# One of 257 dimensions as an outer product on VectorE in place of a matmul, in a Fourier and two-MLP kernel

## The chip, the core and the metric

The kernel runs on one NeuronCore of a Trainium2 chip. The metric is the device time of one execution in microseconds (us). Its engines are called PE (TensorE, the matmuls), DVE (VectorE), ACT (ScalarE), POOL (GpSimd) and SP (SyncE, which issues most DMAs here). Each works through its own queue in order, and they meet at semaphores. Only PE writes matmul results; they go to PSUM, eight banks of 512 fp32 words per partition, which DVE and ACT read.

## What is computed

A two-dimensional Fourier transform over sequence and feature dimension, of which the real part is kept, then an MLP with squared ReLU, then one with a rational function:

```python
X = np.fft.fft(np.fft.fft(x, axis=1), axis=2).real      # x: 2 x 3008 x 256
x = X.reshape(6016, 256)
h = x @ w_in                                            # 256 x 2048
g = np.maximum(h, 0.0) ** 2
x = g @ w_out                                           # 2048 x 256
h = x @ w_in2
P = a[0] + a[1] * h + a[2] * h**2 + a[3] * h**3
Q = 1.0 + abs(b[0]) * abs(h) + abs(b[1]) * h**2
out = (P / (Q + 1e-06)) @ w_out2
```

## The kernel before

**Symmetry.** The input is real, so token k and token -k share their work. With the feature transform folded into w_in, h of token k is plus + minus and h of token -k is plus - minus. Plus needs 129 input dimensions (0 to 128) and minus 127, while a matmul takes 128. Plus has therefore one dimension too many, number 128, and minus one row free: the values of dimension 128 lie in row 0 of the second half (`y[...][0, 1, :]`), and the weights that belong to them in row 0 of the second half of the folded w_in.

**Precision.** Every fp32 value is split in a hi and a lo part (fp32r), and a product is three matmuls: lo of the weights by hi of the data, hi by lo, hi by hi. Dimension 128 takes a fourth matmul in plus (L828): `w_mid` and `y_mid` are full 128-row tiles of zeros with three rows set (hi, hi and lo of one operand against lo, hi and hi of the other), so that one matmul holds all three products.

**Stages.** Stage 1 (L745) is the first Fourier step; w_in is folded (L754), ACT keeps its hi (L478) and DVE its lo (L636). Stage 3 (L765) gives y, the transform of 256 token pairs at a time, in 12 tiles; ACT and DVE keep y_hi (L483) and y_lo (L640), SP stores them in DRAM and loads one tile at a time later (L363, with y_mid at L367). Ten of the 12 tiles are made before the main loop (`EARLY`), two in its first steps.

**The main loop.** A tile (256 pairs, 512 tokens; 196 pairs in the last) takes eight steps, each of two blocks of 128 of the 2048 hidden units; there are 96 steps. In step s PE does up1(s), that is minus (L817, six matmuls of 256 columns) and plus (L828, eight), then down1(s-2) (L802, twelve of 512 columns), up2(s-10) (L793, twelve) and down2(s-12) (L802, twelve). So the first ten steps have no second MLP, and steps behind the last up1 (from about 974 us) have only it.

- ACT in a step: relu and square (L501, L503), once a tile z_hi (L557), from h2 (L519, L527), the hi of g1 (L510), once a tile out_s (L564), abs of q (L533), the copy of minus for step s+1 (L495), ln and exp for a first reciprocal (L543, L546).
- DVE in a step: h = plus + minus and plus - minus (L658, L659), in the first eleven steps the lo of g1 (`split1`, L697), the division for the step before (L676, L678, L682), once a tile z_lo (`keep_z_lo`, L687), then from h2 (`read_h2`: L665, L666, L668). L665 waits for ACT's L527 of the same step. The next up2 on PE waits for L668 (`h2_read`), since both use the same two banks.
- POOL splits the weights w_out1, w_in2 and w_out2 (L421, L423; the last two at about 88 to 122 us), and from step 10 the g values (L446, L453, L455).

Plus stands in PSUM bank 0, minus in bank 1. PE's up1(m) waits for `diff_done` m, after which both banks are read.

## Time and profile before

| | |
|---|---|
| median of 3 runs | 1050.05 us (1049.68 to 1050.45) |
| profiled execution | 1051.58 us, span 1049.8 us |
| busy | PE 97%, DVE 84%, ACT 85%, POOL 54% |
| chain that ended last | PE 89%, DVE 6%, issue 3%, ACT 2% |
| mean granted TensorE clock | 0.989 of full speed |

Busy is the share of the span in which an engine had an instruction running; a matmul's length in a row includes the tail that overlaps the next, so the distance between starts is its price. A granted clock of 1.00 is 2.4 GHz and 0.50 is 1.2 GHz. A row of a timeline gives start and length in us, then engine, line, operation, output<-input and shapes; in brackets the idle time before it and what ended it.

### The profile page before, as it was taken

The page shows a single profiled execution, that of the slowest core. Times are in us where ns is not written, and L with a number is a line of the kernel's source. Part 1 is how long each engine was busy: PE and PEld are TensorE (multiplying, and loading weights), DVE is VectorE, ACT ScalarE, POOL GpSimd, SP SyncE. Part 2 cuts the span into 40 slices and gives each one's busy share as a digit, 9 for nine tenths or more (in the row PEclk, how much of TensorE's full clock was granted, in tenths as well). Part 3 has the DMA queues.
Part 4 walks back from the last instruction along what each step waited for, and adds up shares of the span by engine and source line. Part 5 has one row for each costly group of instructions (what it writes and reads, how often), then busy time and mean ns, then how long its engine had stood idle before and what let it go on. Part 6 is the DMA issues. An engine that isn't in the chain of part 4 may idle for free.

```text
span 1049.8 us, 13876 instructions
## 1 busy us (share of the span) xinstructions
PE 1021.1 (97%) x5288; PEld 868.6 (83%) x5288; DVE 884.0 (84%) x839; ACT 888.6 (85%) x929; POOL 570.6 (54%) x303
## 2 busy tenths in 40 slices
PE   9999999999999999999999999999999999999786
PEld 8798878888888888888888888888888888888675
DVE  2456888988988988888888888898898898898897
ACT  2348888999999999999999999999999998898683
POOL 0236765565665655655656556556566466466442
PEclk9999999999999999999999999999999999999897
DMA  9765000001001001001001001001001001000000
GB/s 249 282 205 193 1 1 21 1 1 41 1 1 42 1 1 41 1 1 41 2 1 41 1 1 41 1 1 41 1 1 41 1 1 36 1 21 2 0 21 16
DMA packets 22580, 36.50 MB, mean 35 GB/s; under 512 B 1601, under 2 KB 17394, under 8 KB 21874
## 3 DMA queue, kind: packets, MB, share of 16 engines
q1 hardware_dynamic: 22514, 35.63, 10.4%
q8 instruction: 41, 0.67, 0.3%
q14 instruction: 25, 0.20, 0.1%
HBM read 23.78 MB, written 11.81 MB: 34 GB/s over the span
## 4 chain that ended last, share of the span: by engine, by line
PE 89%; DVE 6%; issue 3%; ACT 2%; DMA 0%; SPq 0%; ACTq 0%; DVEq 0%
PE ps L802 45%; PE ps L793 23%; PE ps L828 8%; PE ps L817 6%; PE ps L745 3%; PE ps L765 2%; PE ps L754 1%; DVE w_out_unsplit_lo L665 1%; DVE den_s L665 1%; DVE w_out_unsplit_lo L678 1%; DVE w_out_unsplit_lo L676 1%; PE ps L772 1%; DVE w_in_unsplit_hi L666 1%; ACT g_value L527 0%; DVE w_in_unsplit_lo L666 0%
## 5 line engine op out<-in xcount | busy, mean ns | idle before, releaser
L802 PE MATMUL ps<-g_hi,w_out_lo 128*128 128x512 f32 (+1 forms) x764 | 300.9, 394 | 19.8 <-POOL w_in_hi L455 8.9
L802 PE MATMUL ps<-g_hi,w_out_hi 128*128 128x512 f32 (+1 forms) x764 | 299.9, 393 | 0.0
L802 PE MATMUL ps<-g_lo,w_out_hi 128*128 128x512 f32 (+1 forms) x728 | 283.3, 389 | 0.0
L453 POOL CAST g_hi<-g_value 128x1024 fp32r<-128x1024 f32 x86 | 89.7, 1043 | 349.1 <-DVE g_value L682 349.1
L455 POOL TENSOR_TENSOR g_lo<-g_value,g_hi 128x1024 fp32r<-128x1024 f32 x86 | 207.9, 2417 | 6.9
L446 POOL TENSOR_TENSOR g_lo<-g_value,g_hi 128x1024 fp32r<-128x1024 f32 (+1 forms) x86 | 203.8, 2370 | 1.3 <-ACT g_hi L510 1.3
L802 PEld LDWEIGHTS ps<-g_hi,w_out_lo 128*128 128x128 f32 x764 | 145.5, 190 | 49.4 <-POOL w_in_lo L455 10.2
L802 PEld LDWEIGHTS ps<-g_hi,w_out_hi 128*128 128x128 f32 x764 | 145.1, 190 | 29.3
L665 DVE SCALAR_TENSOR_TENSOR den_s<-den_s,b_abs,ps 128x1024 f32<-128x1024 f32 x88 | 112.7, 1281 | 62.4 <-ACT g_value L527 62.1
L802 PEld LDWEIGHTS ps<-g_lo,w_out_hi 128*128 128x128 f32 x728 | 137.6, 189 | 25.5
L676 DVE SCALAR_TENSOR_TENSOR den_s<-den_s,seed_s 128x1024 f32<-128x1024 f32 x87 | 110.9, 1275 | 28.7 <-ACT seed_s L546 28.7
L533 ACT ACTIVATE den_s<-den_s 128x1024 f32<-128x1024 f32 x88 | 93.5, 1063 | 38.4 <-DVE den_s L665 38.3
L793 PE MATMUL ps<-z_hi,w_in_lo 128*128 128x512 f32 (+1 forms) x384 | 118.8, 390 | 2.9 <-DVE g_value L668 2.7
L519 ACT ACTIVATE den_s<-ps,coef_s 128x1024 f32<-128x1024 f32 x88 | 98.2, 1116 | 24.4 <-PE ps L793 23.0
L793 PE MATMUL ps<-z_lo,w_in_hi 128*128 128x512 f32 (+1 forms) x384 | 117.5, 387 | 0.0
L793 PE MATMUL ps<-z_hi,w_in_hi 128*128 128x512 f32 (+1 forms) x384 | 117.3, 387 | 0.0
L682 DVE SCALAR_TENSOR_TENSOR g_value<-g_value,coef_s,den_s 128x1024 f32<-128x1024 f32 x86 | 110.5, 1285 | 3.0
L668 DVE SCALAR_TENSOR_TENSOR g_value<-g_value,coef_s,ps 128x1024 f32<-128x1024 f32 x86 | 110.1, 1281 | 3.0
L678 DVE SCALAR_TENSOR_TENSOR den_s<-den_s,seed_s 128x1024 f32<-128x1024 f32 x87 | 106.6, 1225 | 3.0
L501 ACT ACTIVATE g_value<-g_value 128x1024 f32<-128x1024 f32 (+1 forms) x96 | 100.1, 1042 | 8.2 <-DVE g_value L659 8.2
L666 DVE TENSOR_TENSOR g_value<-g_value,ps 128x1024 f32<-128x1024 f32 x86 | 104.4, 1214 | 0.0
L527 ACT ACTIVATE g_value<-ps,coef_s 128x1024 f32<-128x1024 f32 x86 | 103.3, 1201 | 0.0
(99 smaller groups left out, 1882.8 us busy)
## 6 DMA issues: line engine op xcount, KB each, us to landing
x_s<-x SPq DMA_DIRECT2D x16, 384.0 KB, 7.0
out_t<-out_s SPq DMA_DIRECT2D x11, 512.0 KB, 3.1
w_out_unsplit_lo<-w_out SPq DMA_DIRECT2D x2, 2048.0 KB, 18.2
tw_s<-twiddle SPq DMA_DIRECT2D x1, 3012.0 KB, 17.8
y_hi_dram<-y_stage_hi SPq DMA_DIRECT2D x10, 256.0 KB, 3.2
y_lo_dram<-y_stage_lo SPq DMA_DIRECT2D x10, 256.0 KB, 3.5
y_hi<-y_hi_dram SPq DMA_DIRECT2D x10, 256.0 KB, 2.8
y_lo<-y_lo_dram SPq DMA_DIRECT2D x10, 256.0 KB, 3.1
```

The lines of the kernel that those rows point to most:

```text
L446: nc.gpsimd.tensor_tensor(g1_lo_s[:, p, :, 0:n], r_s[:, p, :, 0:n], g1_hi_s[:, m % 2, :, 0:n].bitcast(F32), ALU.subtract).then_inc(pool_lo ...
L455: nc.gpsimd.tensor_tensor(lo, g, hi.bitcast(F32), ALU.subtract).then_inc(g2_lo, 1)
L501: nc.scalar.activation(r, r, ACT.Relu).then_inc(relu_done, 1)
L527: nc.scalar.activation(num_of(m), h2_banks(m)[:, :, 0:width(m)], ACT.Identity, bias=a2, scale=a3).then_inc(cubic_done, 1)
L665: nc.vector.scalar_tensor_tensor(den, den, b_abs[:, 0:1], h2, ALU.add, ALU.mult).then_inc(q_signed, 1)
L666: nc.vector.tensor_tensor(num, num, h2, ALU.mult).then_inc(t_h_done, 1)
L668: nc.vector.scalar_tensor_tensor(num, num, a1, h2, ALU.add, ALU.mult).then_inc(h2_read, 1)
L676: nc.vector.scalar_tensor_tensor(den, den, Q_CONST, seed, ALU.add, ALU.mult).then_inc(t_done, 1)
L678: nc.vector.scalar_tensor_tensor(den, den, 2.0, seed, ALU.subtract, ALU.mult, reverse0=True).then_inc(rec_done, 1)
L682: nc.vector.scalar_tensor_tensor(num, num, a0, den, ALU.add, ALU.mult).then_inc(g2_done, 1)
L793: last = nc.tensor.matmul(h[:, i, 0:n], lhs, rhs, start=(j == 0), stop=(j == len(products) - 1))
L802: last = nc.tensor.matmul(acc[:, mb, 0:n], w[a][:, f, mb * P:(mb + 1) * P], g[c][:, i, 0:n], start=(f == 0 and j == 0), stop=(f == FB - 1 ...
```

## The change

Dimension 128 leaves the matmuls of plus. DVE writes the outer product of its 256 y values (the same row in all partitions, `u_s`) and its 128 weights (one per partition, a column of `w_col`) into bank 0, two instructions per step with `tensor_scalar`, and PE's six remaining matmuls of plus accumulate on it (`start=False` throughout). `outer_product(s + 1)` stands in DVE's step s behind the division and z_lo and ahead of `read_h2`; the first stands ahead of the loop. PE's plus waits for `outer_ready`, two per step. PE's minus now waits for `minus_kept` where up1 waited for `diff_done`.

For the operands: the row of y is copied by DVE from PSUM with each y_lo (`u_stage`, ahead of the y_lo subtraction), stored in DRAM by SP and loaded by SP into all partitions, in two buffers a tile ahead. The weight row goes from SBUF to DRAM (SP) and back as 32 rows (ACT issues that load at the fourth early tile); PE adds hi and lo and turns them to columns with one small matmul behind the ten early stages 3, and DVE copies the result. The memsets of `w_mid` and `y_mid`, the three DMAs of `w_mid` and three per tile of `y_mid` are gone.

```diff
@@ SP
+            after(sp, s1_ready, S1_GROUPS)
+            sp.dma_start(pair_s[:, :], pair).then_inc(pair_loaded, 16)
-            def load_mid(t, hi, lo):
-                for row, v in enumerate((hi, hi, lo)):
-                    sp.dma_start(y_mid[row:row + 1, 0:pairs(t)].bitcast(F32), v).then_inc(y_mid_loaded, 16)
+            def store_u(t):
+                n = t % (STAGE_BUFS + 1)
+                sp.wait_ge(u_kept, t + 1)
+                sp.dma_start(u_d[:, t * WIDE:t * WIDE + pairs(t)], u_stage[:, n, 0:pairs(t)]).then_inc(u_stored[n], 16)
+
+            def load_u(t):
+                n = pairs(t)
+                after_u_stored(sp, t)
+                sp.dma_start(u_s[:, t % U_BUFS, 0:n], u_d[:, t * WIDE:t * WIDE + n].to_broadcast([P, n])
+                             ).then_inc(u_loaded[t % U_BUFS], 16)
-            sp.wait_ge(mid_zeroed, 2)
             sp.wait_ge(w_in1_lo, folds)
-            for row, n in enumerate((1, 0, 0)):
-                sp.dma_start(w_mid[row:row + 1, :].bitcast(F32), w_in1_s[n][0:1, 1, :].bitcast(F32)).then_inc(w_mid_loaded, 16)
-            sp.wait_ge(y_lo_kept, 1)
-            load_mid(0, *(s[0:1, 1, :].bitcast(F32) for s in y_s))
+            for n in range(2):
+                sp.dma_start(w_row_d[n:n + 1, :], w_in1_s[n][0:1, 1, :].bitcast(F32)).then_inc(w_row_stored, 16)
+            store_u(0)
             for t in range(1, TILES):
+                store_u(t)
                 store_y(t)
+                if t <= U_BUFS:
+                    load_u(t - 1)
@@ SP, main loop
                 load_y(t)
-                load_mid(t, *(v[0:1, 1, t * WIDE:t * WIDE + pairs(t)] for v in y_d))
+                if t + 1 < TILES and t + 1 >= U_BUFS:
+                    load_u(t + 1)
@@ ACT
             for t in range(EARLY):
                 keep_y_hi(t)
+                if t == MID_AT:
+                    act.wait_ge(w_row_stored, 32)
+                    act.dma_start(w_rows[:, :], w_row_d.rearrange("n (f p) -> (n f) p", p=P)).then_inc(w_rows_loaded, 16)
@@ DVE
-            dve.memset(w_mid[:, :].bitcast(F32), 0.0).then_inc(mid_zeroed, 1)
-            dve.memset(y_mid[:, :].bitcast(F32), 0.0).then_inc(mid_zeroed, 1)
             def keep_y_lo(t):
                 hi, lo = y_tile(t)
                 dve.wait_ge(y_hi_kept, t + 1)
+                if t > STAGE_BUFS:
+                    after_u_stored(dve, t - STAGE_BUFS - 1)
+                nc.vector.tensor_copy(u_stage[:, t % (STAGE_BUFS + 1), 0:pairs(t)], uv_bank(t)[0:1, 1, :]).then_inc(u_kept, 1)
@@
                 if t == MID_AT:
-                    dve.wait_ge(w_mid_loaded, 48)
+                    dve.wait_ge(w_row_stored, 32)
@@
+            dve.wait_ge(w_col_summed, 1)
+            nc.vector.tensor_copy(w_col[:, :], ps[:, FOLD_BANKS[2], 0:FB]).then_inc(w_col_ready, 1)
+            dve.wait_ge(w_col_ready, 1)
+
+            def outer_product(m):
+                t, n = m // UNITS, pairs(m // UNITS)
+                if m % UNITS == 0:
+                    dve.wait_ge(u_loaded[t % U_BUFS], 16 * (t // U_BUFS + 1))
+                after(dve, diff_done, m)
+                for i in range(2):
+                    f = 2 * (m % UNITS) + i
+                    nc.vector.tensor_scalar(h1_plus(m)[:, i, :], u_s[:, t % U_BUFS, 0:n], w_col[:, f:f + 1], None, ALU.mult
+                                            ).then_inc(outer_ready, 1)
@@
+            outer_product(0)
             for s in range(STEPS):
@@
                     keep_z_lo(summed // UNITS)
+                if unit(s + 1) is not None:
+                    outer_product(s + 1)
                 if second is not None:
                     read_h2(second)
@@ PE
             for t in range(EARLY):
                 stage3(t)
+            pe.wait_ge(pair_loaded, 16)
+            pe.wait_ge(w_rows_loaded, 16)
+            nc.tensor.matmul(ps[:, FOLD_BANKS[2], 0:FB], w_rows[:, :], pair_s[:, :], start=True, stop=True
+                             ).then_inc(w_col_summed, 1)
@@ PE, up1
-                after(pe, diff_done, m)
+                after(pe, minus_kept, m)
@@
-                if m % UNITS == 0:
-                    pe.wait_ge(y_mid_loaded, 48 * (t + 1))
+                pe.wait_ge(outer_ready, 2 * m + 2)
                 for i in range(2):
                     f = slice((2 * (m % UNITS) + i) * P, (2 * (m % UNITS) + i + 1) * P)
-                    products = [(w_in1_s[1][:, 0, f], y_s[0][:, 0, 0:n]), (w_in1_s[0][:, 0, f], y_s[1][:, 0, 0:n]),
-                                (w_mid[:, f], y_mid[:, 0:n]), (w_in1_s[0][:, 0, f], y_s[0][:, 0, 0:n])]
-                    for j, (lhs, rhs) in enumerate(products):
-                        last = nc.tensor.matmul(h1_plus(m)[:, i, :], lhs, rhs, start=(i == 0 and j == 0), stop=(j == 3),
-                                                skip_group_check=True)
+                    for a, c in ((1, 0), (0, 1), (0, 0)):
+                        last = nc.tensor.matmul(h1_plus(m)[:, i, :], w_in1_s[a][:, 0, f], y_s[c][:, 0, 0:n],
+                                                start=False, stop=(a, c) == (0, 0), skip_group_check=True)
```

## Rows read from the trace of the kernel before

**Rows 1.** Busy time by stretch: stretch, length, PE PEld DVE ACT POOL, clock, DMA, GB/s.
```profile
350.30:429.90 79.60, 79.58 (x402) 67.37 (x401) 70.39 (x66) 73.20 (x75) 46.66 (x24) 1.00 0.04 14
906.00:974.00 68.00, 67.17 (x358) 59.12 (x357) 60.60 (x57) 59.51 (x64) 37.69 (x22) 1.00 0.02 9
```

**Rows 2.** Chain that ended last, in order of time: start, us, what.
```profile
113.73 0.95 PE ps L828 x8
...
145.17 4.41 PE ps L793 x12
...
355.99 2.98 PE ps L793 x12
...
435.63 3.00 PE ps L793 x12
...
950.23 2.74 PE ps L793 x12
...
959.38 2.74 PE ps L793 x12
```

**Rows 3.** Timeline of DVE, one step of the steady part.
```profile
401.02 1.28 DVE L665 SCALAR_TENSOR_TENSOR den_s<-den_s,b_abs,ps 128x1024 f32<-128x1024 f32 x1 [0.91 <-ACT g_value L527]
...
403.47 1.28 DVE L668 SCALAR_TENSOR_TENSOR g_value<-g_value,coef_s,ps 128x1024 f32<-128x1024 f32 x1
404.67 0.68 DVE L658 TENSOR_TENSOR g_value<-ps,minus_s 128x512 f32<-128x512 f32 x1
405.27 0.68 DVE L659 TENSOR_TENSOR g_value<-ps,minus_s 128x512 f32<-128x512 f32 x1
406.22 1.23 DVE L676 SCALAR_TENSOR_TENSOR den_s<-den_s,seed_s 128x1024 f32<-128x1024 f32 x1 [0.27 <-ACT seed_s L546]
...
408.75 1.28 DVE L682 SCALAR_TENSOR_TENSOR g_value<-g_value,coef_s,den_s 128x1024 f32<-128x1024 f32 x1
410.94 1.28 DVE L665 SCALAR_TENSOR_TENSOR den_s<-den_s,b_abs,ps 128x1024 f32<-128x1024 f32 x1 [0.91 <-ACT g_value L527]
```

**Rows 4.** Timeline of PE, the first matmul of plus and the first behind it.
```profile
401.94 0.28 PE L828 MATMUL ps<-y_hi,w_in_lo 128*128 128x256 f32 x1
...
402.88 0.39 PE L802 MATMUL ps<-g_hi,w_out_lo 128*128 128x512 f32 x1
```

**Rows 5.** Timeline of ACT in the same step.
```profile
402.34 1.06 ACT L533 ACTIVATE den_s<-den_s 128x1024 f32<-128x1024 f32 x1 [0.49 <-DVE den_s L665]
```

**Rows 6.** Timeline of DVE, z_lo and the operation behind it.
```profile
114.33 1.23 DVE L687 TENSOR_TENSOR z_lo<-ps,z_hi 128x1024 fp32r<-128x1024 f32 x1
115.47 0.68 DVE L658 TENSOR_TENSOR g_value<-ps,minus_s 128x512 f32<-128x512 f32 x1
```

**Rows 7.** Timeline of DVE at the start of the main loop.
```profile
68.51 0.69 DVE L640 TENSOR_TENSOR y_stage_lo<-ps,y_stage_hi 128x512 fp32r<-128x512 f32 x1 [1.10 <-ACT y_stage_hi L483]
...
75.84 1.23 DVE L697 TENSOR_TENSOR g_lo<-g_value,g_hi 128x1024 fp32r<-128x1024 f32 x1
76.98 0.56 DVE L640 TENSOR_TENSOR y_stage_lo<-ps,y_stage_hi 128x392 fp32r<-128x392 f32 x1
```

**Rows 8.** Timeline of PE, first matmul of plus in steps 0 and 2.
```profile
68.39 0.28 PE L828 MATMUL ps<-y_hi,w_in_lo 128*128 128x256 f32 x1
...
76.06 0.28 PE L828 MATMUL ps<-y_hi,w_in_lo 128*128 128x256 f32 x1
```

**Rows 9.** Instructions of L697 (split1): length in ns min/median/max, first and last start.
```profile
L697 DVE TENSOR_TENSOR g_lo<-g_value,g_hi x10: 1212/1855/3323, 75.8 to 116.7; 128x1024 fp32r<-128x1024 f32 x10
```

**Rows 10.** Timeline of PE, the longest idle time of the first 900 us.
```profile
145.17 0.73 PE L793 MATMUL ps<-z_hi,w_in_lo 128*128 128x512 f32 x2 [1.91 <-DVE g_value L668]
```

**Rows 11.** Busy time of PE by stretch, shortly after: stretch, length, PE, clock, DMA, GB/s.
```profile
147.00:149.00 2.00, 2.00 (x7) 0.50 0.00 0
```

**Rows 12.** Timeline of DVE, L665 in steps 10 and 11.
```profile
122.61 1.28 DVE L665 SCALAR_TENSOR_TENSOR den_s<-den_s,b_abs,ps 128x1024 f32<-128x1024 f32 x1 [3.75 <-ACT g_value L527]
...
132.00 1.28 DVE L665 SCALAR_TENSOR_TENSOR den_s<-den_s,b_abs,ps 128x1024 f32<-128x1024 f32 x1 [0.40 <-ACT g_value L527]
```

More of the change, by code:

```diff
@@ L48 @@
 MID_AT = 3
+U_BUFS = 2
 WIDE = 2 * BATCH * N2
@@ L179, in kept_and_rest @@
             return value, sb(f"{name}_lo", [P, bufs, 2, TN], F32R)
-        w_mid = sb("w_mid", [P, DFF], F32R)
-        y_mid = sb("y_mid", [P, WIDE], F32R)
+        u_s = sb("u_s", [P, U_BUFS, WIDE])
+        w_rows = sb("w_rows", [2 * FB, P])
+        pair_s = sb("pair_s", [2 * FB, FB])
+        w_col = sb("w_col", [P, FB])
+        u_stage = sb("u_stage", [1, STAGE_BUFS + 1, WIDE])
+        sb("to_w_in2", [P, DFF + WIDE - (U_BUFS + STAGE_BUFS + 1) * WIDE - P - 2 * FB])
         w_in2_s, (_, w_in2_raw) = weights("w_in2", [P, DB, DFF])
@@ L875, in _ @@
             pe.wait_ge(w_in1_lo, folds)
-            pe.wait_ge(w_mid_loaded, 48)
             pe.wait_ge(mid_row_zeroed, 2)
```

17 lines of the change are left out of this document (13 added, 4 removed).

## The prediction

> **What bounds the kernel now.** I read the table of busy time by stretch first. From 350.3 to 429.9 us, one tile of eight steps, PE is busy for 79.58 of 79.60 us at full clock, DVE for 70.39 and ACT for 73.20; the last h1 tile (906 to 974) looks alike [rows 1]. So PE sets the pace, and a tile lasts 435.63 - 355.99 = 79.64 us [rows 2]. Matmuls taken off PE shorten the time only until another engine comes last, so what counts is how near DVE is. The timeline of one step shows it: DVE's L665 starts at 401.02 and again at 410.94, a step of 9.92 us, and DVE is idle twice in it, 0.27 us before L676 and 0.91 us before L665, both times for ACT [rows 3]. The new DVE work falls just into the 0.91.
>
> **PE's side.** In plus the eight matmuls (L828) take 402.88 - 401.94 = 0.94 us, 0.118 each [rows 4]. Two fewer per step is -0.236: a step needs 9.68 us of PE, a tile 79.64 - 1.89 = 77.75. The 96 steps hold 22.6 us of it, the most the change can give.
>
> **What a product costs DVE.** No row of before shows DVE writing PSUM, nor this operation. Nearest rows: L658, 512 columns, gives way to L659 after 0.60 us, that is 512 columns at 1.04 ns (from 512 to 1024 columns an element costs (1.28 - 0.68)/512 to 1.04 ns depending on form) plus 0.07. L668, with a per-partition scalar read from memory, is 1.28 long and gives way after 1.20 = 1.07 + 0.13; L676, whose scalars are constants, is only 1.23 long [rows 3]. The product reads such a scalar (a column of w_col), so I take 0.27 + 0.13 = 0.40 us of DVE per product of 256 columns and 0.48 to its end: 0.80 per step, 0.88 until PE may go on. Lower bound 0.27 (two elements at a time, the same 0.13), middle 0.34 (scalar for nothing), upper 0.50 (a dearer write to PSUM).
>
> By the Trainium skill, "VectorE: DVE Perf Modes", section "The TRN2 errata", a lone fp32 operation of N elements takes (N+151)/0.96 ns, an estimate of 424 ns here; less the 0.08 overlap that would be the 0.34 of the first rival. The trace agrees with it for L658 (0.68) and not for the forms with a scalar from memory (1.28 for 1024, where it gives 1.22).
>
> **The steady loop.** L665 starts, ACT's L533 follows 1.32 later, then L495, L543 and L546, whose end releases DVE's L676 at 406.22 [rows 3, 5]: 5.20 us. L676 and L678 take 408.75 - 406.22 = 2.53 together, and L682 gives way after 1.20, as L668 does: 8.93. In before the next L665 then waits for L527. In after, outer_product(s+1) stands there: 8.93 + 0.80 = 9.73, above PE's 9.68. The 0.91 cover is used up. Once a tile z_lo (L687) stands in this place as well. It gives way after 115.47 - 114.33 = 1.14 us [rows 6], so this step takes 10.87. A tile: 8 x 9.73 + 1.14, and 0.2 for ACT's out_s and for POOL overlap (estimate) = 79.1. The gain per tile is 0.5 and not 1.89. From 152 to 906 us are 9.5 tiles: **-4.5 us** (at 0.27: -18, PE-bound; at 0.34: -14.5; at 0.50, the loop at 9.93: +10).
> What is late next: PE's plus of the step after z_lo waits for outer_ready about 1 us. Queued behind it on PE are down1, up2 and down2, for which ACT and DVE wait; since the loop is DVE's, that wait is the same time seen on PE.
>
> **The last h1 tile.** With 196 columns a product is 0.34, and the loop 5.1 (a narrower L495) + 3.73 + 0.67 = 9.5, against steps of 959.38 - 950.23 = 9.15 [rows 2]. Seven steps: **+2**.
>
> **The first ten steps.** There is no h2 work here; a step of PE is up1 and down1. Three things come on:
> (a) outer_product(0). The product of step 0 must wait for PE's w_col matmul, which itself stands behind the last early stage 3, for the y_lo copy that starts at 68.51 [rows 7] and now has a row copy of u before it (0.34), for a copy of w_col (about 0.2) and for itself (0.88): 70.5. Its plus started at 68.39 [rows 8]: 2.1 us later.
> (b) step 2. On DVE in step 1 come y_lo(10), split1(0) at 75.84, y_lo(11) at 76.98 [rows 7] and only then outer_product(2). Two u copies add 0.6, the end of y_lo(11) is near 78.1, the product 79.0, and with the delay of (a) passed on less 0.24 and some slack 80.5. Plus(2) ran at 76.06 [rows 8]: +4.4. PE is in order, so down1(0) is late by the same.
> (c) a new loop through steps 3 to 10: plus(s) 0.71 and 0.2 to its reader, add and subtract 1.20, split1(s-1), outer_product(s+1) 0.88, plus(s+1): 2.98 plus the length of split1. That length goes from 1.21 (median 1.86) to 3.32 us [rows 9], long while POOL splits the second weights. So I take 4.2, 4.2, 4.5, 4.75, 5.0, 5.0, then 6.3, and 7.4 with z_lo behind the last: 41.4 us from plus(2) to plus(10). Before it was 113.73 - 76.06 = 37.67 [rows 2, 8]: +3.7.
> Together +8.1, less 0.2 for the shorter plus(10): **+7.9**. Bounds 4 (POOL's splits end before the late steps, slack in step 1) and 10.
> (d) the clock. After an idle time of 1.91 us at 145.17 the granted clock of the stretch 147 to 149 is 0.50, the 1.2 GHz level [rows 10, 11]; the twelve matmuls took 4.41 where 2.74 is usual [rows 2], 1.67 lost. Waits of over 2 us will stand ahead of plus(0), plus(2) and plus(10). Three times 1.67 less what is hidden: **+3.5**, bounds 0 and 5.
> (e) steps 10 to 12 are paced by the loop of ACT and DVE already, at 132.00 - 122.61 = 9.39 us [rows 12]: 9.73 makes **+1**.
>
> **At nothing.** The two memsets and the 39 small DMAs (3 of w_mid, 36 of y_mid) that go lie beside waits of others. Added on SP: two stores of w_row, twelve stores and twelve loads of u, and pair. The loads of u are a tile ahead, so a landing has most of a tile, 80 us, as cover; without that DVE's product would wait for it once a tile. The first u and the way of w_row through DRAM start with the first early tiles and have until 68, some 10 us. The u stores stand before y's stores on SP, a short issue each; the load of w_in2 follows y_lo(11), some 2 us later, and POOL's splits with it. On ACT the load of w_rows waits for w_row_stored at step 3 of the early tiles and may hold up y_hi a little. PE's minus now waits for minus_kept, earlier than diff_done. The tail after 974 us, DVE's chain, isn't touched and only starts later.
>
> **Sum.** -4.5 + 2 + 7.9 + 3.5 + 1 = +9.9 us. The profiled execution took 1051.58 (span 1049.8), 1.5 above the median of 1050.05; added to the median this is **1060**.
>
> **Rivals.**
> First: a product costs 0.34. Then a tile takes 8 x 9.60 + 1.3 = 78.1: -14.5, last tile +1, head 7 + 3.5 + 0.5: -2.5, about 1047.5. For it: plain forms cost 0.07 beyond their elements. Against: every form here with a scalar from memory is dearer. 0.2.
> Second: DVE has room and PE stays the bound (a product of 0.27 or less), as the change says. -18, +0.5, +6.5 and +3: -8, 1042. The row that speaks for it is DVE's 70.39 of 79.60 busy; against it speaks the loop through ACT, which busy shares don't show. 0.1.
> Third: the head loses little, since the waits of steps 1 to 10 overlap others, at 0.40 per product: -4.5 + 2 + 1 and 3: 1051.5, the same. 0.1.
> Fourth, slower still: the wait of about 1 us behind z_lo is enough to halve the clock each tile. 1.67 lost, 0.7 of it hidden, 9.5 times 1: 1069.5. It decides from where idle is as long as the 1.91 us there [rows 10]. 0.1.
> The forecast has 0.5.
>
> **How the numbers follow.** 0.2% (2.1 us) is about what a measurement can tell from no change. Faster is the second rival and most of the first; no change is the third and the rest of the first; slower the forecast and the fourth: 0.25, 0.15, 0.6. The range leaves out the tip of either side: 1044 to 1068; the forecast's own, from its bounds, is 1053 to 1067.
>
> **What would show it.** Products of 0.48 us each, giving way after 0.40; L665 in steady steps behind outer_product and not behind L527; steps of 9.7; PE idle once a tile ahead of plus; plus(0) near 70.5, plus(2) near 80.5, plus(10) near 122; a clock of 0.5 in parts of 70 to 90. The forecast is wrong if products take 0.35, if PE is still busy without gaps past 152 us, or if plus(10) comes before 118.

## The result

The changed kernel takes 1053.88 us (median of 8 runs, 1052.88 to 1055.89), the kernel before 1050.65 (8 runs), a ratio of 1.0029 with an interval of 1.0020 to 1.0038. It is slower by 3.2 us; the forecast was slower by about 10.

| | before | after |
|---|---|---|
| profiled execution, span | 1051.58, 1049.8 us | 1054.85, 1053.1 us |
| first matmul of minus, step 0 | 67.60 | 67.61 |
| read_h2 of step 10 | 122.61 | 134.00 |
| second z_lo | 190.88 | 203.04 |
| last but one z_lo | 907.46 | 910.56 |
| last z_lo | 975.84 | 980.12 |
| busy | PE 97%, DVE 84%, ACT 85%, POOL 54% | PE 96%, DVE 89%, ACT 84%, POOL 54% |

The table says where the time went: 11.4 us are lost ahead of step 10 and 0.8 up to the second z_lo, 9.1 come back between the second and the last but one z_lo (907.46 - 190.88 = 716.58, now 707.52), 1.2 are lost in the last h1 tile and 1.0 comes back behind it: 3.3 in the two spans. In the kernel after, line numbers have moved: L665, L666 and L668 of read_h2 are L709, L710 and L712 now, L676, L678 and L682 of the division L720, L722 and L726, z_lo is L731, split1 L741, the products are L693, and on PE plus is L876, minus L868, down L853, up2 L844, stage 3 L812. DVE's subtract is L703. On ACT L524 keeps minus, L572 and L575 are the ln and the exp ahead of the division, L556 is the second of the two that read h2, L586 is z_hi.

The page of after: busy time, and the chain that ended last by engine and by line.

```profile
PE 1009.3 (96%) x5098; PEld 852.9 (81%) x5098; DVE 941.7 (89%) x1042; ACT 882.0 (84%) x929; POOL 569.5 (54%) x303
DVE 45%; ACT 28%; issue 14%; PE 12%; DMA 0%; DVEq 0%; ACTq 0%; SPq 0%
```

PE's share of the chain went from 89% to 12% while its busy share fell by one point only. The steady stretch of [rows 1], of after, and two from the start (stretch, length, busy of PE PEld DVE ACT POOL, clock, DMA, GB/s):

```profile
67.50:115.50 48.00, 42.56 (x231) 36.95 (x231) 32.18 (x53) 32.77 (x39) 23.49 (x12) 0.89 0.48 164
115.50:152.00 36.50, 28.75 (x128) 23.83 (x127) 25.41 (x31) 26.31 (x28) 17.73 (x9) 0.86 0.00 0
350.30:429.90 79.60, 78.99 (x390) 66.39 (x389) 76.58 (x84) 73.45 (x76) 47.11 (x25) 1.00 0.05 16
```

In the steady stretch PE is idle 0.6 us of 79.60, and no more. That another path is nevertheless a bound is seen in the chain, here one step of it (start, us, what):

```profile
408.70 1.28 DVE g_value L726
409.99 0.79 DVE ps L693 x2
410.77 1.20 DVE den_s L709
...
412.96 0.58 ACT minus_s L524
413.54 1.05 ACT seed_s L572
...
414.61 1.17 ACT seed_s L575
...
415.87 1.24 DVE den_s L720
417.13 1.24 DVE den_s L722
418.39 0.03 DVE g_value L726
```

From L726 to L726 it is a closed loop through DVE and ACT with no matmul in it, and the two products lie in it. Its length is 418.39 - 408.70 = 9.69 us. The timeline of DVE shows the same step as [rows 3]:

```profile
409.90 0.87 DVE L693 TENSOR_SCALAR ps<-u_s,w_col 128x256 f32<-128x256 f32 x2
410.68 1.27 DVE L709 SCALAR_TENSOR_TENSOR den_s<-den_s,b_abs,ps 128x1024 f32<-128x1024 f32 x1
...
415.87 1.23 DVE L720 SCALAR_TENSOR_TENSOR den_s<-den_s,seed_s 128x1024 f32<-128x1024 f32 x1 [0.27 <-ACT seed_s L575]
...
420.38 1.27 DVE L709 SCALAR_TENSOR_TENSOR den_s<-den_s,b_abs,ps 128x1024 f32<-128x1024 f32 x1
```

The 0.91 us ahead of L665 have gone and the 0.27 ahead of the division have stayed. The pair of products gives way after 410.68 - 409.90 = 0.78. In this tile (351 to 430 us) the distances of L709 are seven times 9.68 to 9.70 and, in the step with z_lo, 10.81; 7 x 9.69 + 10.82 is the usual tile of 78.65. PE's wait for the products over the whole steady part (in total, times, longest) is small, one per tile, behind z_lo:

```profile
PE ps L876 <- DVE ps L693: 5.4, 9, 0.7
```

The start, on PE: first matmuls of plus in steps 0, 2 and 10, and stage 3 behind the first.

```profile
70.08 0.38 PE L876 MATMUL ps<-y_hi,w_in_lo 128*128 128x256 f32 x1 [1.50 <-DVE ps L693]
...
71.27 3.16 PE L812 MATMUL ps<-tw_s,s_s 128*128 128x128 f32 x16
...
81.52 0.58 PE L876 MATMUL ps<-y_hi,w_in_lo 128*128 128x256 f32 x1 [3.16 <-DVE ps L693]
...
123.58 0.38 PE L876 MATMUL ps<-y_hi,w_in_lo 128*128 128x256 f32 x1 [3.08 <-DVE ps L693]
```

Plus of step 0 is 1.7 us later than in [rows 8], plus of step 2 is 5.5 later, plus of step 10 10.0 later than the 113.56 at which the timeline of before has it. ([rows 2] show 113.73 for it, but that row is of the chain, where a group of matmuls begins when the tail of the one ahead has ended.) In front of the last one ACT and DVE did this (ACT first):

```profile
120.48 1.00 ACT L586 ACTIVATE z_hi<-ps 128x1024 fp32r<-128x1024 f32 x1
```
```profile
121.52 1.22 DVE L731 TENSOR_TENSOR z_lo<-ps,z_hi 128x1024 fp32r<-128x1024 f32 x1 [2.01 <-ACT z_hi L586]
122.66 0.86 DVE L693 TENSOR_SCALAR ps<-u_s,w_col 128x256 f32<-128x256 f32 x2
```

ACT's z_hi needs the sums of PE's down1, whose last matmul ends at 119.78, and stands in ACT's queue behind the relu and square of step 9, which came from PE's plus and end at 120.58. DVE's z_lo waits 2.01 us for z_hi, the product of step 10 is queued behind z_lo, and PE's plus waits 3.08 us for the product. A product whose place is behind an operation that waits for PE's results makes PE wait for itself. And behind this wait the twelve matmuls of down1 took 4.34 us where the twelve of up2 behind them take 2.77; the chain has them, and the clock of the stretch is 0.50:

```profile
124.56 4.34 PE ps L853 x12
128.89 2.77 PE ps L844 x12
```
```profile
125.50:127.50 2.00, 2.00 (x6) 1.53 (x5) 2.00 (x4) 1.49 (x2) 0.00 (x0) 0.50 0.00 0
```

PE's longest wait for a product, 4.51 us ahead of plus at 143.84, comes behind this part, and the clock is 0.50 from 143 to 147 us. It costs nothing of its own here: from L709 at 134.00 to L709 at 164.70 the chain has no matmul, only DVE and ACT.

### The profile page after: what moved, and what is told of

Same layout as the page of the kernel before. It is cut to its first block, busy times and chain, and to the rows that moved or that the text cites. A ratio compares the mean times of both kernels' runs of the same rounds, so it can differ in the third digit from the quotient of the medians.

```text
span 1053.1 us, 13706 instructions
## 1 busy us (share of the span) xinstructions
PE 1009.3 (96%) x5098; PEld 852.9 (81%) x5098; DVE 941.7 (89%) x1042; ACT 882.0 (84%) x929; POOL 569.5 (54%) x303
## 4 chain that ended last, share of the span: by engine, by line
DVE 45%; ACT 28%; issue 14%; PE 12%; DMA 0%; DVEq 0%; ACTq 0%; SPq 0%
ACT seed_s L575 9%; DVE den_s L709 9%; DVE den_s L722 9%; DVE den_s L720 9%; ACT seed_s L572 8%; DVE g_value L726 8%; ACT minus_s L524 5%; DVE ps L693 4%; PE ps L853 3%; PE ps L792 3%; PE ps L812 2%; PE ps L801 1%; ACT g_value L556 1%; DVE z_lo L731 1%; PE ps L844 1%
## 5 line engine op out<-in xcount | busy, mean ns | idle before, releaser
L853 PE MATMUL ps<-g_hi,w_out_lo 128*128 128x512 f32 (+1 forms) x764 | 302.2, 396 | 18.1 <-POOL w_in_hi L481 8.2
L853 PE MATMUL ps<-g_hi,w_out_hi 128*128 128x512 f32 (+1 forms) x764 | 301.3, 394 | 0.0
L853 PE MATMUL ps<-g_lo,w_out_hi 128*128 128x512 f32 (+1 forms) x728 | 285.3, 392 | 0.0
L853 PEld LDWEIGHTS ps<-g_hi,w_out_lo 128*128 128x128 f32 x764 | 146.9, 192 | 47.0 <-POOL w_in_lo L481 9.5
L853 PEld LDWEIGHTS ps<-g_hi,w_out_hi 128*128 128x128 f32 x764 | 146.3, 191 | 29.8
L853 PEld LDWEIGHTS ps<-g_lo,w_out_hi 128*128 128x128 f32 x728 | 138.8, 191 | 25.9
L720 DVE SCALAR_TENSOR_TENSOR den_s<-den_s,seed_s 128x1024 f32<-128x1024 f32 x87 | 106.8, 1228 | 25.5 <-ACT seed_s L575 25.5
L844 PE MATMUL ps<-z_hi,w_in_lo 128*128 128x512 f32 (+1 forms) x384 | 118.9, 391 | 1.8 <-DVE g_value L712 1.8
L709 DVE SCALAR_TENSOR_TENSOR den_s<-den_s,b_abs,ps 128x1024 f32<-128x1024 f32 x88 | 111.9, 1272 | 8.6 <-ACT g_value L556 8.3
L844 PE MATMUL ps<-z_lo,w_in_hi 128*128 128x512 f32 (+1 forms) x384 | 117.2, 386 | 0.0
L844 PE MATMUL ps<-z_hi,w_in_hi 128*128 128x512 f32 (+1 forms) x384 | 116.9, 386 | 0.0
L726 DVE SCALAR_TENSOR_TENSOR g_value<-g_value,coef_s,den_s 128x1024 f32<-128x1024 f32 x86 | 110.5, 1284 | 3.0
L712 DVE SCALAR_TENSOR_TENSOR g_value<-g_value,coef_s,ps 128x1024 f32<-128x1024 f32 x86 | 110.2, 1281 | 3.0
L722 DVE SCALAR_TENSOR_TENSOR den_s<-den_s,seed_s 128x1024 f32<-128x1024 f32 x87 | 106.6, 1225 | 3.0
L710 DVE TENSOR_TENSOR g_value<-g_value,ps 128x1024 f32<-128x1024 f32 x86 | 104.3, 1213 | 0.0
L556 ACT ACTIVATE g_value<-ps,coef_s 128x1024 f32<-128x1024 f32 x86 | 103.1, 1198 | 0.0
```

What stands on the lines that cost most here:

```text
L556: nc.scalar.activation(num_of(m), h2_banks(m)[:, :, 0:width(m)], ACT.Identity, bias=a2, scale=a3).then_inc(cubic_done, 1)
L709: nc.vector.scalar_tensor_tensor(den, den, b_abs[:, 0:1], h2, ALU.add, ALU.mult).then_inc(q_signed, 1)
L710: nc.vector.tensor_tensor(num, num, h2, ALU.mult).then_inc(t_h_done, 1)
L712: nc.vector.scalar_tensor_tensor(num, num, a1, h2, ALU.add, ALU.mult).then_inc(h2_read, 1)
L720: nc.vector.scalar_tensor_tensor(den, den, Q_CONST, seed, ALU.add, ALU.mult).then_inc(t_done, 1)
L722: nc.vector.scalar_tensor_tensor(den, den, 2.0, seed, ALU.subtract, ALU.mult, reverse0=True).then_inc(rec_done, 1)
```

## The experiments

Unless it says otherwise an experiment is an edit of the changed kernel. Ratios are to the kernel before, run on the same chip; that kernel's median was 1051.17 beside e1, e2, e3 and e4_head_place, 1050.16 beside e4b to e7 and 1051.20 beside e8 to e12. The diffs show the lines that matter and not each line of an edit. Head means the time from the first matmul of minus(0) to read_h2 of step 10: 55.01 us before, 66.39 after. Tile is the usual distance of two z_lo in the steady part: 79.64 before, 78.65 after. Last is the distance of the last two z_lo: 68.38 before, 69.56 after.

| | median us | ratio (95%) | head | tile | last |
|---|---|---|---|---|---|
| e1_six_matmuls | 1034.11 | 0.9838 (0.9824 to 0.9853) | 52.57 | 78.06 | 67.95 |
| e2_constant_scalar | 1048.98 | 0.9978 (0.9969 to 0.9988) | 65.70 | 78.18 | 68.88 |
| e9_four_halves | 1076.95 | 1.0246 (1.0226 to 1.0266) | 65.73 | 80.54 | 71.01 |
| e5_eight_matmuls | 1067.35 | 1.0165 (1.0149 to 1.0180) | 67.84 | 79.72 | 69.79 |
| e3_early_place | 1038.62 | 0.9882 (0.9867 to 0.9897) | 57.96 | 78.07 | 67.89 |
| e4_head_place | 1044.84 | 0.9945 (0.9930 to 0.9960) | 56.57 | 78.65 | 69.54 |
| e4b_steady_place | 1047.39 | 0.9972 (0.9961 to 0.9983) | 66.46 | 78.06 | 67.96 |
| e8_step1_only | 1050.20 | 0.9993 (0.9984 to 1.0003) | 61.22 | 78.65 | 69.58 |
| e11_early_column | 1051.40 | 1.0007 (0.9998 to 1.0017) | 64.18 | 78.65 | 69.55 |
| e6_filler | 1051.54 | 1.0013 (1.0003 to 1.0024) | 60.70 | 78.65 | 69.58 |
| e12_changed_again | 1054.03 | 1.0030 (1.0018 to 1.0041) | 64.92 | 78.65 | 69.58 |
| e7_both_ends | 1033.81 | 0.9845 (0.9831 to 0.9860) | 53.27 | 78.06 | 67.96 |

### What the shorter PE alone is worth

An edit of the kernel before: the matmul of w_mid and y_mid is left out and nothing takes its place, so dimension 128 is missing from h of the first layer.

```diff
-                                (w_mid[:, f], y_mid[:, 0:n]), (w_in1_s[0][:, 0, f], y_s[0][:, 0, 0:n])]
+                                (w_in1_s[0][:, 0, f], y_s[0][:, 0, 0:n])]
```

> The PE half of the change alone: the kernel before without its fourth matmul in plus, so dimension 128 is left out of the first MLP, and with no product on DVE. Theory (PE sets the pace before the change, and DVE's product is what takes the gain back): the full saving of 0.236 us per step appears, a tile goes from 79.64 to 77.75, L665 stays behind L527, the head gains about 2 us and the last tile 1.5: 1050.6 - 22 = 1029 us. Rival (PE was not the only bound, another loop holds the step near 9.7): a tile stays near 78.6 and the time near 1040.

Measured: 17.1 us faster, not the 22.6 of the 192 matmuls. The tile is 78.06 and not 77.75, and the last tile 67.95, only 0.43 shorter. PE's waits between 160 and 900 us, a kind that the kernel before doesn't have there:

```profile
PE ps L793 <- DVE g_value L668: 3.3, 10, 1.0
```

That is 0.33 us per tile, 0.25 in most: in the step with z_lo up2 waits for DVE's read_h2, and this is most of the 78.06 - 77.75. So even without a product PE isn't alone in setting the pace, and the ceiling of the change lay at 17 us; the 1029 us expected were too low, and a tile of 78.6 as the rival had it didn't come. PE's own step without the two matmuls is seen here too, from the starts of minus in three steps (z_lo comes between the last two):

```profile
413.57 0.28 PE L817 MATMUL ps<-y_hi,w_in_lo 128*128 128x256 f32 x1
...
423.26 0.28 PE L817 MATMUL ps<-y_hi,w_in_lo 128*128 128x256 f32 x1
...
433.44 0.28 PE L817 MATMUL ps<-y_hi,w_in_lo 128*128 128x256 f32 x1
```

The usual step is 9.69 and the one with z_lo 10.18. The usual step of the changed kernel is 9.69 as well. So the products cost nothing in seven steps of eight, and what after lacks against this ceiling, 78.65 - 78.06, stands in the step with z_lo alone, 10.82 against 10.18. In the last tile the steps keep the length that they had before; PE's busy 67.17 of 68.00 [rows 1] had looked like a bound and wasn't one.

### How long the loop is

Three kernels change the DVE work in the loop, or PE's, by a known amount. In the first the column of w_col is a constant, so that dimension 128 has wrong weights:

```diff
-                    nc.vector.tensor_scalar(h1_plus(m)[:, i, :], u_s[:, t % U_BUFS, 0:n], w_col[:, f:f + 1], None, ALU.mult
+                    nc.vector.tensor_scalar(h1_plus(m)[:, i, :], u_s[:, t % U_BUFS, 0:n], 0.5, None, ALU.mult
```

> The changed kernel with the constant 0.5 in place of the column of w_col, so dimension 128 has wrong weights; place and number of the products are unchanged. Theory (the loop L709, L524, L572, L575, L720, L722, L726, two products sets the steady step at 9.69; a scalar from memory costs 0.06 us): a product gives way after 0.33 instead of 0.39, the loop falls to 9.57, below PE's 9.68, a tile goes from 78.65 to between 77.8 and 78.1, the last tile gains 1: 1045 to 1047 us. Rival 1 (the scalar costs nothing): products and time as in the changed kernel, 1053.9. Rival 2 (PE's handshake with DVE, not the length of the loop, holds the step): product shorter, but tile still 78.6.

DVE of this kernel:

```profile
427.04 0.75 DVE L693 TENSOR_SCALAR ps<-u_s 128x256 f32<-128x256 f32 x2
427.69 1.27 DVE L709 SCALAR_TENSOR_TENSOR den_s<-den_s,b_abs,ps 128x1024 f32<-128x1024 f32 x1
...
432.88 1.31 DVE L720 SCALAR_TENSOR_TENSOR den_s<-den_s,seed_s 128x1024 f32<-128x1024 f32 x1 [0.27 <-ACT seed_s L575]
```

The pair gives way after 0.65 instead of 0.78, a product after 0.33: the scalar from memory costs 0.06 each. DVE's steps went to 9.64 only, since L720 takes 1.31 here instead of 1.23 and so takes 0.08 of the 0.13 back; behind z_lo it takes 1.23, and there the step is 9.57. (When this L720 starts, a subtraction of POOL that began at 430.68 still has 0.23 us to run; in after it is 0.10. The last section comes back to this.) PE's steps stay at 9.69, their length without any product, except in the step with z_lo, where they went from 10.75 to 10.33: DVE, now a little faster than PE in the usual steps, makes up for part of z_lo there. The tile is 78.18 and not 78.1 or less, the time 1048.98 and not 1045 to 1047 as expected. A product of 0.33 is the first rival's price, and its tile was 78.1.

In the second each product is made in two halves:

```diff
-                    nc.vector.tensor_scalar(h1_plus(m)[:, i, :], u_s[:, t % U_BUFS, 0:n], w_col[:, f:f + 1], None, ALU.mult
-                                            ).then_inc(outer_ready, 1)
+                    for part in (slice(0, n // 2), slice(n // 2, n)):
+                        nc.vector.tensor_scalar(h1_plus(m)[:, i, part], u_s[:, t % U_BUFS, part], w_col[:, f:f + 1], None, ALU.mult
+                                                ).then_inc(outer_ready, 1)
@@ PE
-                pe.wait_ge(outer_ready, 2 * m + 2)
+                pe.wait_ge(outer_ready, 4 * m + 4)
```

> The changed kernel with each product written as two halves of 128 columns, so four short instructions a step in the same place; nothing is left out. Theory (the loop through DVE and ACT is the steady step, to the last tenth): a half gives way after 0.25 us (0.13 for its elements and 0.12 fixed, the rest of 0.39), four take 1.02 instead of 0.78, a step goes from 9.69 to 9.93 and a tile from 78.65 to 80.6: +18 in the steady part, +1.7 in the last tile, +2 in the head: 1076. Rival (the step is set by something else with slack for DVE of 0.2 us or more): 1056 or less.

```profile
435.50 1.11 DVE L694 TENSOR_SCALAR ps<-u_s,w_col 128x128 f32<-128x128 f32 x4
436.52 1.27 DVE L710 SCALAR_TENSOR_TENSOR den_s<-den_s,b_abs,ps 128x1024 f32<-128x1024 f32 x1
```

The four give way after 1.02, which is 0.24 more than the pair, and a step is 9.93, 0.24 more than 9.69; the tile is 1.89 longer, about eight times 0.24. What is added to DVE in this place is added to the step in full: the loop has no slack left. What is taken off does not all come back, as e2_constant_scalar showed, since PE's own step is as long.

In the third the hi by lo matmul is issued twice per block, so its product counts twice, and PE has eight matmuls in plus again:

```diff
-                    for a, c in ((1, 0), (0, 1), (0, 0)):
+                    for a, c in ((1, 0), (0, 1), (0, 1), (0, 0)):
```

> The DVE half of the change alone: the changed kernel with two matmuls per step more in plus (w_hi by y_lo twice, so that term counts double), which gives PE its old 9.92 us per step. Theory: DVE's loop of 9.69 lies below PE's 9.92, so the products cost nothing in steady steps: tiles of 79.6 to 79.7 as in the kernel before, no wait of PE for L693 there. The head keeps its loss and adds PE's 0.24 per step: L709 of step 10 near 135.5. The last tile (loop 9.46 against PE's 9.15) loses 1.2. Sum: 1050.7 + 13 = 1064. Rival (DVE's writes to PSUM or the handshake slow PE by themselves): tiles above 80 and 1068 or more.

The steady stretch of this kernel:

```profile
350.30:429.90 79.60, 79.60 (x401) 67.49 (x400) 76.11 (x81) 73.14 (x74) 46.66 (x24) 1.00 0.05 16
```

PE is busy throughout, waits for nothing between 160 and 900 us, and the tile is 79.72 against 79.64 before. At PE's step of 9.93 the products are free. How z_lo is paid for is seen in L709, here behind a step with z_lo of 10.90:

```profile
366.02 1.28 DVE L709 SCALAR_TENSOR_TENSOR den_s<-den_s,b_abs,ps 128x1024 f32<-128x1024 f32 x1
...
375.72 1.27 DVE L709 SCALAR_TENSOR_TENSOR den_s<-den_s,b_abs,ps 128x1024 f32<-128x1024 f32 x1
```

The next steps of DVE are 9.70, 9.69, 9.77 and 9.85 and then PE's 9.93 again: the loop runs at its own 9.69 until it has made up for z_lo. In after it can't, since PE's step has come down to the loop's. So the change gained PE's 0.23 in the usual steps and lost the cover for z_lo: 79.64 - 78.65 = 0.99 per tile in place of 1.89. Of the 17 us that this kernel is slower than before, 12.8 are the head and 1.4 the last tile; 1064 was expected.

### The place of the products

The products of step s+1 need that add and subtract of step s have read bank 0, and nothing else that is late. In the next kernel they stand directly behind it.

```diff
                 add_and_subtract(s)
+                if unit(s + 1) is not None:
+                    outer_product(s + 1)
...
-                if unit(s + 1) is not None:
-                    outer_product(s + 1)
                 if second is not None:
                     read_h2(second)
```

> The changed kernel with outer_product(s+1) directly behind add_and_subtract(s) in every step, where DVE waits 0.27 us for L575 anyway; nothing is left out. Theory (loops): in steady steps the pair hides 0.27 us and costs 0.5 to 0.6 in the loop, which falls to 9.4 to 9.5, below PE's 9.68: tile 77.75 to 77.9, L709 behind L556 again. In the head the product no longer stands behind split1, y_lo and z_lo: plus(2) near 78 instead of 81.5, one halving of the clock less, L709 of step 10 at 124 to 126 instead of 134.0. Together 1050.6 + 2.5 - 18 - 2 = 1033 us. Rival (DVE is simply full, 76.6 of 78.65 us busy per tile, or PE pays for accumulating on a bank that DVE wrote): a tile stays within 0.3 of 78.65, and only the head's part of 8 to 9 us comes: 1045.

```profile
433.26 0.68 DVE L703 TENSOR_TENSOR g_value<-ps,minus_s 128x512 f32<-128x512 f32 x1
433.98 0.87 DVE L693 TENSOR_SCALAR ps<-u_s,w_col 128x256 f32<-128x256 f32 x2
434.76 1.22 DVE L720 SCALAR_TENSOR_TENSOR den_s<-den_s,seed_s 128x1024 f32<-128x1024 f32 x1
...
437.27 1.28 DVE L726 SCALAR_TENSOR_TENSOR g_value<-g_value,coef_s,den_s 128x1024 f32<-128x1024 f32 x1
438.47 1.28 DVE L709 SCALAR_TENSOR_TENSOR den_s<-den_s,b_abs,ps 128x1024 f32<-128x1024 f32 x1
```

The products now begin in the gap in which the division waited for ACT, so 0.27 of them is free, L709 stands directly behind L726, and this step behind z_lo is 9.45. In the others L720 takes up to 1.42 and a step of DVE is about 9.65, still under PE's 9.69. A tile is 78.07, the same as in e1_six_matmuls, where there is no product at all. The kernel is faster than before by 1.2%, 12.6 us; 1033 us had been expected, from tiles of 77.75 to 77.9 that e1_six_matmuls doesn't reach either. The next two make this move in the first ten steps only, and from step 10 on only (the diff of the first; the second has the two conditions the other way round):

```diff
+                if s < SKEW:
+                    outer_product(s + 1)
...
-                if unit(s + 1) is not None:
+                if s >= SKEW and unit(s + 1) is not None:
                     outer_product(s + 1)
```

> The changed kernel with the product directly behind add_and_subtract in steps 0 to 9 only; from step 10 on it stands where the changed kernel has it. Theory (the head costs 11.4 us by the start of the second MLP, of which 1.7 are the late first product and 8 to 10 the place of the others and the clock they cost): L709 of step 10 at 124 to 126, tiles 78.65 as in the changed kernel: 1044 to 1046 us. Rival (the head's delay is made up later in any case, since the chain's later parts have slack): the time stays at 1053, with the tail or the tiles longer.

> The changed kernel with the product directly behind add_and_subtract from step 10 on, and in its old place before. Theory: the steady part and the last tile gain what e3 gained there, 0.59 per tile (78.65 to 78.06) and 1.3: 5.4 + 1.3 less 0.9 that the tail gave back = 1048. L709 of step 10 near 134 as in the changed kernel. Rival (the head's lag and the steady loop interact): tiles near 78.65 again.

Each against the kernel before on its own chip, the head alone is at -6.3 us, the steady part alone at -2.8 and both at -12.6, where the changed kernel is at +3.2. So the moves gave 9.6, 6.0 and 15.8, and the parts add up (15.6). Beside the 6.0 stand 0.59 per tile over some nine tiles and 1.6 in the last h1 tile; beside the 9.6 a head that is 9.8 shorter.

### What the head is made of

First the product of step 2 alone, the only one placed early:

```diff
+                if s == 1:
+                    outer_product(s + 1)
...
-                if unit(s + 1) is not None:
+                if s != 1 and unit(s + 1) is not None:
                     outer_product(s + 1)
```

> The changed kernel with only the product of step 2 moved: in DVE's step 1 it stands directly behind add_and_subtract, ahead of y_lo(10), split1(0) and y_lo(11). Theory: plus(2) starts near 78.3 instead of 81.5 and the clock isn't halved in 81 to 85 us, so L709 of step 10 comes at 129 instead of 134.0, and the time is 1049.5. The other 4 to 5 us that e4 gained are then those of steps 3 to 10, behind split1 and z_lo. Rival (all of it belongs to steps 3 to 10): L709 of step 10 at 133 or later, 1053.

Then the other cause at the start, the late w_col. PE's matmul for it stands behind the eighth of the ten early stages 3, and DVE's copy and the product of step 0 behind the eighth y_lo; all else is as in after:

```diff
+COL_AT = 7
...
@@ DVE, behind keep_y_lo(t) of the early tiles
+                if t == COL_AT:
+                    dve.wait_ge(w_col_summed, 1)
+                    nc.vector.tensor_copy(w_col[:, :], ps[:, FOLD_BANKS[2], 0:FB]).then_inc(w_col_ready, 1)
+                    dve.wait_ge(w_col_ready, 1)
+                    outer_product(0)
@@ PE, behind stage3(t)
+                if t == COL_AT:
+                    pe.wait_ge(pair_loaded, 16)
+                    pe.wait_ge(w_rows_loaded, 16)
+                    nc.tensor.matmul(ps[:, FOLD_BANKS[2], 0:FB], w_rows[:, :], pair_s[:, :], start=True, stop=True
+                                     ).then_inc(w_col_summed, 1)
```

> The changed kernel with only the start moved: the w_col matmul behind the eighth early stage 3, its copy and the product of step 0 behind y_lo(7). Theory: plus(0) at 68.2 instead of 70.1 and no halved clock in 71 to 73 us, so everything to step 10 comes 1.7 to 3.3 us earlier, L709 of step 10 at 131 to 132, time 1051. Rival (step 2's wait takes it up): L709 of step 10 at 134, time 1053.9.

And the changed kernel once more beside these two:

> The changed kernel unchanged, beside the others on the same chip, as the measure for them and for how far two executions differ in the head. Every theory: 1053 to 1055, L709 of step 10 at 133 to 135, tiles 78.65.

Against the changed kernel on the same chip (1054.03, head 64.92), the early product of step 2 alone gives 3.8 us (head -3.7) and the early w_col alone 2.6 us, with a head only 0.7 shorter, though plus(0) starts 0.79 us behind minus(0) as before and not 2.47 as in after; the profiled execution of e11_early_column (1053.67) is the slowest of its ten, so its median is the better witness. The rest of the head, from e8_step1_only's 61.22 to e4_head_place's 56.57, is 4.7 us: the products of steps 3 to 10, which stood behind split1 and, in step 10, behind z_lo. e8_step1_only still has PE's 3.08 us of idle time ahead of plus(10), while in e4_head_place no wait for a product is over 0.5 us from plus(1) to plus(10). How the rest is shared among the other steps isn't shown.

### The clock

The idle times of 1.50 and 3.16 us in the head are followed in after by the lower level of the clock, as in [rows 10, 11]. Here 11 and 22 extra matmuls into an unused bank fill them, so that PE isn't idle; they take nothing from what follows them unless they are too many; of the two idle times 0.17 and 0.67 us are left.

```diff
                 last.then_inc(minus_ready, 1)
+                for _ in range({0: 11, 2: 22}.get(m, 0)):
+                    nc.tensor.matmul(ps[:, FOLD_BANKS[3], 0:WIDE], w_in1_s[0][:, 0, 0:P], y_s[0][:, 0, :], start=True, stop=True)
                 pe.wait_ge(outer_ready, 2 * m + 2)
```

> The changed kernel with 11 matmuls of 256 columns into an unused bank ahead of PE's wait for the products of step 0 and 22 ahead of that of step 2, so that PE isn't idle there. Theory (these two idle times of 1.5 and 3.2 us halve the granted clock, 0.50 in 71 to 73 and 81 to 85 us, and that costs 3 us): clock 1.00 through 68 to 90, the sixteen stage 3 matmuls behind plus(0) take 1.8 instead of 3.4 us, L709 of step 10 at 131 instead of 134.0, time 1051. Rival (the clock's loss lies beside other waits): clock 1.00 but L709 of step 10 stays at 134 and the time at 1053.9.

PE of this kernel; then PE of e12_changed_again, that is of after in another execution; then the clock between 71 and 73 us in after, in this kernel and in e12_changed_again.

```profile
68.99 1.48 PE L873 MATMUL ps<-y_hi,w_in_hi 128*128 128x256 f32 x11
70.65 0.39 PE L878 MATMUL ps<-y_hi,w_in_lo 128*128 128x256 f32 x1 [0.17 <-DVE ps L693]
...
71.47 1.95 PE L812 MATMUL ps<-tw_s,s_s 128*128 128x128 f32 x16
```
```profile
70.84 0.39 PE L876 MATMUL ps<-y_hi,w_in_lo 128*128 128x256 f32 x1 [1.50 <-DVE ps L693]
...
71.66 1.95 PE L812 MATMUL ps<-tw_s,s_s 128*128 128x128 f32 x16
...
80.89 0.39 PE L876 MATMUL ps<-y_hi,w_in_lo 128*128 128x256 f32 x1 [3.31 <-DVE ps L693]
...
82.17 0.62 PE L853 MATMUL ps<-g_hi,w_out_hi 128*128 128x512 f32 x1
```
```profile
71.00:73.00 2.00, 2.00 (x12) 2.00 (x11) 1.46 (x3) 0.11 (x1) 0.00 (x0) 0.50 1.11 332
```
```profile
71.00:73.00 2.00, 2.00 (x20) 2.00 (x19) 1.30 (x3) 0.00 (x0) 0.00 (x0) 1.00 1.11 340
```
```profile
71.00:73.00 2.00, 2.00 (x19) 2.00 (x20) 1.14 (x2) 0.00 (x0) 0.00 (x0) 1.00 1.11 331
```

With the gaps filled the sixteen matmuls of stage 3 took 1.95 us, in after 3.16. But the same 1.50 us of idle time ahead of them brought the lower level in one execution of the changed kernel and not in the other. And the filled kernel kept the full clock at a place that wasn't filled, ahead of plus(10); here that wait and the eight us behind it:

```profile
119.98 0.39 PE L878 MATMUL ps<-y_hi,w_in_lo 128*128 128x256 f32 x1 [3.09 <-DVE ps L693]
```
```profile
121.00:129.00 8.00, 8.00 (x42) 6.76 (x41) 3.55 (x6) 4.58 (x5) 4.82 (x3) 1.00 0.00 0
```

So the clock's share of the head isn't one number, and the filled kernel's profiled execution owes part of its head to a place without filler. That head is 5.7 us shorter than that of after, while the median is 1.4 us above the kernel before on its chip, where after was 3.2 and e12_changed_again 2.8 above. How much of the 11.4 us a clock that stays up would give back in a typical execution is settled no better than this, from 1.4 to 5.7 us.

### Both together

The early place for all products, as in e3_early_place, and the early w_col, as in e11_early_column:

```diff
+COL_AT = 7
...
                 add_and_subtract(s)
+                if unit(s + 1) is not None:
+                    outer_product(s + 1)
```

> The early place in all steps, and in addition the small matmul for w_col behind the eighth early stage 3 instead of the tenth, with the copy of w_col and the product of step 0 behind y_lo(7) on DVE; nothing is left out. Theory (the late first product costs 1.7 us and one halving of the clock 1.6): plus(0) starts near 68.2 instead of 70.1, clock 1.00 from 68 to 75, L709 of step 10 at 122 to 123, time 1035, near the 1034.1 of the kernel without products. Rival (the start is bound by something else, such as y_lo(9) to (11) or POOL): L709 of step 10 stays at 124 or later, 1038.

PE's waits between 160 and 900 us, and its first matmul of plus, which waits for nothing:

```profile
PE ps L846 <- DVE g_value L714: 3.8, 10, 1.0
```
```profile
68.28 0.28 PE L878 MATMUL ps<-y_hi,w_in_lo 128*128 128x256 f32 x1
```

1033.81 us, 16.3 less than the kernel before on the same chip; e1_six_matmuls, in which the products don't exist, is 17.1 less on its own, and the intervals of the two ratios overlap. PE's only wait in the steady part is the one that e1_six_matmuls has too. The head is 53.27 us, 1.7 shorter than before and 0.7 longer than that of e1_six_matmuls. This is the version to keep: nearly all that the two fewer matmuls can give is there, and the products cost 0.7 us at most.

## Why the prediction was right or wrong, step by step

**The direction and its reason held.** Products of 0.48 that give way after 0.40 were predicted, and 0.48 and 0.39 came. L709 starts behind the products and no longer behind ACT; steps of 9.7 (9.69); PE idle about once a tile ahead of plus; plus(0) 70.08 (70.5), plus(2) 81.52 (80.5), plus(10) 123.58 (122); a clock of 0.50 in parts of 70 to 90. That DVE's loop through ACT would have no room left, though DVE looked 12% idle, is shown by e9_four_halves and e5_eight_matmuls. By the Trainium skill, "Perfetto Trace Analysis", section "Identifying the Most-Contended Engine", the occupancy of DVE is a fair measure of how close one is to its roofline. By that DVE's 76.58 of 79.60 would leave 3 us per tile; here the measurement decides otherwise, for in e9_four_halves 0.24 us of added work cost 0.24, since the 0.27 idle time belongs to the loop.

**The step that failed is the steady loop's sum**, with its 79.1 per tile and -4.5 in all. Measured is 78.65, and -9.7 from step 13 to the last but one z_lo. The mechanism is right but for one point, and its size was off: the rest of the loop is 8.91 and not 8.93 and a pair of products 0.78 and not 0.80, together 0.04 per step; the step with z_lo is 10.82 and not 10.87; and the 0.2 per tile for out_s and POOL's overlap, an estimate, isn't there at all. By 9.5 tiles these are 3 and 2 us. No length in the loop was wrong by more than 3%, but the gain is the difference of 9.92 and 9.73, and an error of 0.04 in it is an error of a fifth. The point: 9.73 stood above PE's 9.68, so the products were to cost something in each step. The loop's 9.69 is PE's own step (e1_six_matmuls), and what the products cost against that ceiling is some 0.6 us in the step with z_lo, which DVE can no longer make up for. The bounds of the product (0.27 to 0.50) did no harm here: the value taken from [rows 3] was right to 0.01. (At 0.34 the loop is 9.61 and not the 9.60 that the first rival takes.) What was missing is a bound on the loop itself.

**The last h1 tile** was sized at +2 and is +1.2. Steps are 9.46 (9.5 predicted), but part of that tile's time isn't in such steps: the tile as a whole grew from 68.38 to 69.56.

**The first ten steps** were sized at 7.9 and 3.5 for the clock, 11.4, and measured 11.39. The sum is right to the second digit and its parts are not. (a) 1.7 instead of 2.1. (b) 5.5 instead of 4.4, since the halved clock behind plus(0) fell into it (stage 3 took 3.16 us instead of 1.95), which (d) had counted. (c) plus(2) to plus(10) is 42.06 us, 4.6 more than the 37.50 of before (3.7 predicted; the 37.67 of the prediction sets a row of the chain against one of the timeline, 0.17 apart), and not by the route predicted: split1, put at up to 3.32 us in the late steps, took 1.57 at most, and in its place stand a step of 6.2 us at the halved clock behind plus(2) (add and subtract from 83.21 to 89.43) and the 3.08 us ahead of plus(10), where the product waits behind z_lo. From plus(10) to L709 come 1.4 us more (10.42, before 9.05), the third halved stretch. The round trip from PE over ACT (z_hi) and DVE (z_lo) back to PE had been noted as one operation in the queue, not as a wait on PE's own results. (d) was three halved stretches, and this execution had all three; e12_changed_again shows that they don't come each time, and its head is 1.5 us shorter. That the total was right to a tenth is luck.

**(e)** steps 10 to 12: +1 predicted, 12.76 - 11.39 = 1.4 measured, from L709 at 164.70 in step 13 against 151.94.

**The tail** was taken as moved only. It is 1.0 us shorter (73.96 to 72.98 from the last z_lo to the end). Experiments with the same code there show 72.9 as well as 73.7 to 74.1, so this is the execution and not the change.

Together, measured against predicted: head 12.8 to 12.4, steady -9.7 to -4.5, last tile 1.2 to 2, tail -1.0 to 0; 3.3 to 9.9.

**The rivals.** The first, a product at 0.34, isn't what happened, but e2_constant_scalar has that price and came out at 1048.98 (1047.5 forecast). The second, PE still the bound, needs a tile of 77.75, and that doesn't exist: without any product it is 78.06. The third fell in the traces, since the head lost 11.4 us, although its 1051.5 was nearer to the measured time than the forecast. The fourth didn't happen: the wait behind z_lo is 0.7 us at most and the clock of the steady stretch is 1.00.

## What to carry over

When work moves from a full engine to one with room, look for the closed loop through the other engines that the new work would lengthen, and measure its length from the trace; the busy share of neither engine shows it (here 0.78 us of work in a loop with 1.01 of room left 0.23 of gain per step, and nothing to cover the 1.1 us that come once a tile). Put such work in the slot where its engine already waits for another one, and never behind an operation that itself waits for the engine that the work feeds: moving two lines turned +3 us into -12.6. And where a forecast is the difference of two loops of almost equal length, state its range as the error of one step times the number of steps.
